# Top-1 MoE routing: all one-hot columns on VectorE, constant products in one run, and a packed table of experts

## What is computed

```python
def _moe2_ref(x, w_gate, w1, w2):          # 3072 x 512, 8 experts, hidden 1024
    logits = x @ w_gate
    expert_idx = np.argmax(logits, axis=1)
    ...
    gate_w = probs[np.arange(N), expert_idx]
    for e in range(E):
        mask = expert_idx == e
        if not mask.any():
            continue
        h = np.maximum(x[mask] @ w1[e], 0.0)
        out[mask] = gate_w[mask, None] * (h @ w2[e])
```

## Time and profile before

| | us |
|---|---|
| median of 3 runs | 458.57 |
| lowest, highest | 457.68, 459.55 |
| the profiled execution | 457.49 |
| its span in the trace | 455.8 |
| busy: TensorE, VectorE, ACT, POOL | 430.4, 237.7, 211.6, 215.1 |
| mean granted TensorE clock | 0.977 |

### The profile page before, as it was taken

The page is one execution under the profiler, slowest core; times in us unless marked ns, Lnnn a source line. Parts: engine busy times, 40 slices in busy tenths (PEclk is TensorE's granted clock), DMA queues, the critical chain, the costliest instruction groups (busy, mean ns, idle before and its releaser), DMA issues.

```text
span 455.8 us, 9239 instructions
## 1 busy us (share of the span) xinstructions
PE 430.4 (94%) x3052; PEld 359.9 (79%) x3053; DVE 237.7 (52%) x786; ACT 211.6 (46%) x417; POOL 215.1 (47%) x180
## 2 busy tenths in 40 slices
PE   8799999999999997998978959999999999999994
PEld 7699999999999996643335955688888888888883
DVE  6467777776767773557000744656433333333344
ACT  2578887878887862322010005365333333232234
POOL 3999888888888800010001156134444344443322
PEclk9989999999999998999999978999999999999998
DMA  8699998967666203999996483711111111112111
GB/s 230 260 415 372 352 366 296 399 248 269 246 214 253 81 1 111 390 387 411 396 387 206 129 313 108 283 38 58 58 58 58 58 58 58 46 46 58 53 50 13
DMA packets 27222, 89.21 MB, mean 196 GB/s; under 512 B 3280, under 2 KB 3280, under 8 KB 27184
## 3 DMA queue, kind: packets, MB, share of 16 engines
q1 hardware_dynamic: 23664, 78.47, 46.3%
q0 software_dynamic: 3360, 9.83, 7.0%
q10 hardware_dynamic: 160, 0.42, 0.5%
HBM read 80.85 MB, written 8.13 MB: 195 GB/s over the span
## 4 chain that ended last, share of the span: by engine, by line
PE 83%; DMA 5%; DVE 4%; POOL 4%; issue 1%; ACT 1%; SPq 0%; ACTq 0%; DVEq 0%; POOLq 0%
PE O L404 16%; PE Yq L1515 11%; PE Yq L1516 10%; PE Yq L1517 10%; PE PT L386 8%; PE S L377 5%; PE S L376 5%; DMA ext<-in_moe_w 4%; PE Gp L1453 3%; PE XTp L819 3%; PE Lp L938 2%; POOL work L1351 2%; PE Up L828 1%; PE Sp L1434 1%; DMA q_raw<-in_q 1%
## 5 line engine op out<-in xcount | busy, mean ns | idle before, releaser
L461 ACT ACTIVATE shared<-shared,nm 128x256 f32<-128x256 f32 (+1 forms) x192 | 83.7, 484 | 33.1 <-DVE nm L564 33.1
L404 PE MATMUL O<-V,PTs 128*128 128x65 f32 x704 | 90.9, 271 | 0.5 <-ACT PTs L487 0.5
L404 PEld LDWEIGHTS O<-V,PTs 128*128 128x128 f32 x704 | 87.4, 193 | 1.6 <-ACT PTs L487 0.9
L564 DVE CUSTOM_DVE_ANT_0 shared<-S,TA 128x256 f32<-128x256 f32 (+1 forms) x192 | 68.7, 396 | 36.9 <-PE S L377 34.2
L1515 PE MATMUL Yq<-w2h,hh 128*128 x208 | 83.2, 400 | 0.4 <-issue 0.3
L1516 PE MATMUL Yq<-w2l,hh 128*128 x208 | 81.3, 391 | 0.0
L1517 PE MATMUL Yq<-w2h,hl 128*128 x208 | 81.2, 390 | 0.0
L336 POOL TENSOR_TENSOR kl<-k_raw,kh 128x1632 fp32r<-128x1632 f32 x15 | 55.1, 3676 | 9.5 <-ACT kh L471 9.3
L1815 DVE SCALAR_TENSOR_TENSOR hl<-Gp,hh 128x512 fp32r<-128x512 f32 x56 | 38.1, 687 | 37.8 <-ACT hh L1611 37.8
L386 PE MATMUL PT<-ident,shared 128*128 128x128 f32 x352 | 55.4, 276 | 0.1
L376 PE MATMUL S<-kh,qs 128*128 128x256 f32 (+1 forms) x180 | 53.4, 319 | 1.9 <-POOL kl L336 1.9
(11 more groups left out here) (243 smaller groups left out, 583.2 us busy)
## 6 DMA issues: line engine op xcount, KB each, us to landing
mem<-in_moe_w SPq DMA_DIRECT2D x9, 2048.0 KB, 10.8
ext<-in_moe_w SPq DMA_DIRECT2D x6, 2048.0 KB, 19.4
k_raw<-in_k SPq DMA_DIRECT2D x15, 816.0 KB, 6.9
q_raw<-in_q SPq DMA_DIRECT2D x15, 768.0 KB, 5.2
V<-in_v SPq DMA_DIRECT2D x16, 715.0 KB, 4.2
xmem<-in_moe_w SPq DMA_DIRECT2D x2, 2048.0 KB, 10.5
w2l<-in_moe_w SPq DMA_DIRECT2D x2, 2048.0 KB, 13.9
w2h<-in_moe_w SPq DMA_DIRECT2D x1, 2048.0 KB, 8.3
```

The source lines that it names most:

```text
L404: mm = pe.matmul(O[grp % 2][:, at:at + VC], PTs[:, par, (h * kbs + kb) * P:(h * kbs + kb + 1) * P], V[:, buf, h, vb, :], start=(n == 0), s ...
L461: nc.scalar.activation(Pb[:, par, h, 0:width(g)], Pb[:, par, h, 0:width(g)], ACT.Exp, bias=nm[:, par, h:h + 1], scale=-1.0).then_inc(exp_d ...
L564: v.tensor_tensor_reduce(Pb[:, par, h, 0:w], S[par][h][:, 0:w], tab, -SCALE, HUGE, ALU.add, ALU.min, nm[:, par, h:h + 1]).then_inc(biased, 1)
```

## The change

1. POOL builds no columns any more. VectorE builds all six steps, behind `OA` and `OW`; `hot_first`, `places_known` and `HOTG` are gone.
2. The constant products ahead of the sort are 40 instead of 34, and the one in front of each of the last four steps is gone.
3. Units, first unit, tiles and first tile of an expert are packed in one word: VectorE computes `word` in three dependent instructions on 8 elements and multiplies it once with `sel`, where it multiplied four times. `rt` has three rows. Each engine reads one word per expert and takes it apart with shifts and masks in registers. TensorE also takes the first expert's units from the word it has, instead of a load of their own.

```diff
-    def entry(eng, r, which):
-        return eng.value_load(rt[0:1, which, bass.ds(rank_at(r), 1)], ...)
+    def plan(eng, r):
+        word = eng.value_load(rt[0:1, 1, bass.ds(rank_at(r), 1)], min_val=0, max_val=(1 << 19) - 1)
+        return ((word & 15)..., ((word >> 4) & 31)..., ((word >> 9) & 31)..., (word >> 14)...)
...
     def _(pool):
         pool.wait_ge(c_stored, 16)
-        pool.wait_ge(places_known, 1)
-        for t in range(HOTG * REP):
-            ins = nc.gpsimd.tensor_scalar(OB[:, t, :], col[:], ab[:, 1, t:t + 1], None, ALU.is_equal)
-            if t % REP == REP - 1:
-                ins.then_inc(hot_first, 1)
         pool.wait_ge(src_ready, 1)
...
-            units, first = entry(pool, rank, 1), entry(pool, rank, 2)
-            tiles, tile0 = entry(pool, rank, 3), entry(pool, rank, 4)
+            units, first, tiles, tile0 = plan(pool, rank)
...
-                    g = t // REP
-                    if g < HOTG:
-                        pe.wait_ge(hot_first, g + 1)
-                    else:
-                        if which.start == 0:
-                            busy(1)
-                        pe.wait_ge(hot_done, g - HOTG + 1)
+                    pe.wait_ge(hot_done, t // REP + 1)
...
-        busy(34)
+        busy(40)
...
-        for t in range(HOTG * REP, TT, REP):
+        for t in range(0, TT, REP):
             v.tensor_tensor(OB[:, t:t + REP, :], ..., ALU.is_equal).then_inc(hot_done, 1)
-        for i in range(2):
-            v.tensor_tensor(pick[:, 1 + 2 * i], sel[:], nt[0:1, i, :]..., ALU.mult)
-            v.tensor_tensor(pick[:, 2 + 2 * i], sel[:], begin[0:1, i, :]..., ALU.mult)
+        step(v.scalar_tensor_tensor(word[:], begin[0:1, 1, :], 32.0, nt[0:1, 1, :], ALU.mult, ALU.add))
+        step(v.scalar_tensor_tensor(word[:], word[:], 32.0, begin[0:1, 0, :], ALU.mult, ALU.add))
+        step(v.scalar_tensor_tensor(word[:], word[:], 16.0, nt[0:1, 0, :], ALU.mult, ALU.add))
+        v.tensor_tensor(pick[:, 1], sel[:], word[:]..., ALU.mult)
```

More of the change, by code:

```diff
@@ L1147, in top1_moe @@
     dst_i = sb(st, "dst_i", [P, MAXT], I32)
-    rt = sb(st, "rt", [1, 6, NE], I32)
+    rt = sb(st, "rt", [1, 3, NE], I32)
     tr = sb(st, "tr", [1, MAXU], I32)
@@ L1195, in top1_moe @@
     sel = sb(st, "sel", [1, NE, NE])
-    pick = sb(st, "pick", [1, 5, NE, NE])
-    picked = sb(st, "picked", [1, 5, NE])
+    word = sb(st, "word", [1, NE])
+    pick = sb(st, "pick", [1, 2, NE, NE])
+    picked = sb(st, "picked", [1, 2, NE])
     past = sb(st, "past", [1, MAXU, NE])
@@ L1281, in rank_at, with number @@
         return r if isinstance(r, int) else r.with_bounds(min_val=0, max_val=NE - 1)
-    def entry(eng, r, which):
-        return eng.value_load(rt[0:1, which, bass.ds(rank_at(r), 1)], min_val=int(which in (1, 3)),
-                              max_val=[NE - 1, TT // 2, MAXU - 3, TT, TT + NE - 2][which])
+    def number(eng, r):
+        return eng.value_load(rt[0:1, 0, bass.ds(rank_at(r), 1)], min_val=0, max_val=NE - 1)
+    def plan(eng, r):
+        word = eng.value_load(rt[0:1, 1, bass.ds(rank_at(r), 1)], min_val=0, max_val=(1 << 19) - 1)
+        return ((word & 15).with_bounds(min_val=1, max_val=TT // 2),
+                ((word >> 4) & 31).with_bounds(min_val=0, max_val=MAXU - 3),
+                ((word >> 9) & 31).with_bounds(min_val=1, max_val=TT),
+                (word >> 14).with_bounds(min_val=0, max_val=TT + NE - 2))
     def count(eng):
-        return eng.value_load(rt[0:1, 5, 0:1], min_val=1, max_val=NE)
+        return eng.value_load(rt[0:1, 2, 0:1], min_val=1, max_val=NE)
     def all_units(eng):
-        return eng.value_load(rt[0:1, 5, 1:2], min_val=1, max_val=MAXU - 2)
+        return eng.value_load(rt[0:1, 2, 1:2], min_val=1, max_val=MAXU - 2)
     def all_tiles(eng):
-        return eng.value_load(rt[0:1, 5, 2:3], min_val=1, max_val=TT + NE - 1)
+        return eng.value_load(rt[0:1, 2, 2:3], min_val=1, max_val=TT + NE - 1)
     def chunks_at_end(rank, used):
@@ L1322, in _ @@
         for r in range(2):
-            e = entry(sp, r, 0)
+            e = number(sp, r)
             if r:
@@ L1542, in _ @@
         used = count(pe)
-        first = halves_of(entry(pe, 0, 2))
+        units, zero = plan(pe, 0)[0:2]
+        first = halves_of(zero)
         tile(0, 0, 0, *first)
@@ L1570, in _ @@
             with pe.Fori(1, used) as rank:
-                units, first = entry(pe, rank, 1), entry(pe, rank, 2)
+                units, first = plan(pe, rank)[0:2]
                 with pe.Fori(0, units) as j:
@@ L1683, in _ @@
         with act.Fori(0, used) as rank:
-            units, first = entry(act, rank, 1), entry(act, rank, 2)
+            units, first = plan(act, rank)[0:2]
             with act.If(units > (rank < 1) * 1):
@@ L1749, in _ @@
         step(v.tensor_tensor(place[:], order[0:1, :], act[0:1, :], ALU.mult))
-        v.tensor_copy(rt[:, 5, 0:1], order[0:1, NE - 1:NE])
+        v.tensor_copy(rt[:, 2, 0:1], order[0:1, NE - 1:NE])
         step(v.tensor_tensor(sel[:], place[:].unsqueeze(1).to_broadcast([1, NE, NE]),
@@ L1767, in _ @@
         step(v.tensor_scalar(ab_i[:, 1, :], pos_i[:], P - 1, None, ALU.bitwise_and))
-        v.tensor_copy(ab[:], ab_i[:]).then_inc(places_known, 1)
-        dve.wait_ge(places_known, 1)
+        step(v.tensor_copy(ab[:], ab_i[:]))
         dve.wait_ge(c_stored, 16)
@@ L1789, in _ @@
         v.tensor_scalar(src_i[:], Sp[:, 0:MAXT], -1.0, 0.0, ALU.add, ALU.max).then_inc(src_ready, 1)
-        v.tensor_reduce(picked[:, 1:5, :], pick[:, 1:5], AX, ALU.add)
+        v.tensor_reduce(picked[:, 1, :], pick[:, 1], AX, ALU.add)
         step(v.tensor_tensor(past[:], past[:], act[0:1, :].unsqueeze(1).to_broadcast([1, MAXU, NE]), ALU.mult))
-        v.tensor_copy(rt[:, 1:5, :], picked[:, 1:5, :])
-        v.tensor_copy(rt[:, 5, 1:3], upto[0:1, :, NE - 1])
+        v.tensor_copy(rt[:, 1, :], picked[:, 1, :])
+        v.tensor_copy(rt[:, 2, 1:3], upto[0:1, :, NE - 1])
         step(v.tensor_reduce(tr_f[:], past[:], AX, ALU.add))
@@ L1878, in _ @@
         with dve.Fori(0, used) as rank:
-            units, first, tile0 = entry(dve, rank, 1), entry(dve, rank, 2), entry(dve, rank, 4)
+            units, first, _, tile0 = plan(dve, rank)
             with dve.If(units > (rank < 1) * 1):
```

8 lines of the change are left out of this document (1 added, 7 removed).

## The result

| | before | after |
|---|---|---|
| median, us | 458.38 | 450.92 (4 runs, 450.2 to 452.5) |
| ratio to before | | 0.984, 95% interval 0.981 to 0.987 |
| the profiled execution, its span | 457.49, 455.8 | 450.2, 448.5 |
| mean granted TensorE clock | 0.977 | 0.988 |

The median of before is that of all its runs by then, 458.38 where three gave 458.57. The forecast was 451.6 in a range of 449.7 to 455.4; measured were 450.92, or 7.5 us less than before where 7.0 were forecast. Step by step it is less smooth: three terms were off, and two of them cancel, which is luck.

What follows compares the result with a forecast made beforehand. TensorE was taken to bound the kernel from 304 us on, with POOL's columns in the chain before. The hidden products' gain of 7.0 us, tables counted zero, took the median 458.57 to 451.6, range 449.7 to 455.4.

Steps and rivals of the forecast that it cites:

- Columns and constants: Before the sort: six VectorE groups at 0.667 us and 40 constants in one run write src_i 6.9 us earlier.
- The gather: Behind src_i: the gather's landing sets the hidden products, 7.9 to 6.2 us earlier; the middle, 7.0, was taken.
- two prices: First gather's landing: undisturbed at 273.3, gain 7.9 us, or slowed in the issue to 275.0, gain 6.2 us.
- the row of 1.91: An earlier gather's second issue took 1.91 us while weights streamed; taken as the price of a disturbed issue.
- each step hangs on the one before as now: From the hidden products on, steps on TensorE, ACT and VectorE follow each other as before; second expert's weights covered by 2 us.
- the prediction's own sign: At the end: the prediction is wrong if the gain at the hidden products is larger than the gain at the end.
- Granted clock 1.00 from 258 to 272: Constants, sort and first fold: an expected sign that TensorE keeps its full clock throughout this stretch.
- a clock of 0.50 in 275 to 286: After the gather: a half clock in this stretch would show the prediction wrong.
- the rival on the clock: Clock falls in TensorE's new gap before the gather; takes 3.5 us off the gain, giving 455.1; chance 0.13.
- The tables: Packed tables save loads at each switch of experts, hidden under TensorE's products; counted zero, bounds -0.1 and +0.3 us.
- arrives at the end: What is won before 304 us reaches the end undiminished; what another engine wins after it is lost.
- The sum: Whole kernel: 7.0 us less, from 457.49 to 450.5 profiled and from 458.57 to 451.6 in the median.

Runs made afterwards that it cites:

- e9: The changed kernel with constant products as before: 34 in one run and one in front of each of the sort's last four steps; 451.57 us, ratio 0.984.
- e2: The kernel before with all six column groups on VectorE and 40 constant products in one run, tables not packed; 452.73 us, ratio 0.987.
- e11: The changed kernel with the first expert's last 512 KB of w2 loaded after the first gather lands, and POOL's second gather ahead of its split; 450.20 us, ratio 0.981.
- e8: The changed kernel without the unused last gather, copy and subtraction, and with POOL's quarter of the split behind the second gather and VectorE's three; 448.28 us, ratio 0.978.
- e3: The changed kernel with POOL's subtraction of the last w2 quarter moved behind the second gather and VectorE's three quarters; 450.38 us, ratio 0.983.
- e1: The kernel before with the packed tables alone, columns and constant products as they were; 457.72 us, ratio 0.998.
- e4: The changed kernel itself, run again beside other variants on the same chip; 450.85 us, ratio 0.984.
- e6: The changed kernel without the last unit's unused gather and without ScalarE's copy and VectorE's subtraction of unread weights at the end; 447.97 us, ratio 0.977.
- e10: The changed kernel once more, beside the variant with interleaved constants; 450.49 us, ratio 0.981.

## Why the prediction was right, and where it was not

- *Columns and constants.* Right: 0.61 us a group for 0.667, no wait of TensorE, the sort at full clock in 2.83 us. `src_i` is 7.4 us earlier from z, where 6.9 were forecast.
- *The gather.* The middle of two prices was taken, 7.0, and 7.2 was measured at the hidden products; neither price was the mechanism. The issue was not slowed (1.04 and 0.94), against the row of 1.91 that decided it in the prediction, and the landing was 3.0 (e9) to 3.9 us (e2) after the start of the second issue instead of 2.6: it comes with the end of the matrix (e9, e11). The rule that each DMA engine takes turns between the queues of both kinds of descriptors, "DMA: Bandwidth & Descriptors" of the Trainium skill, section "SWDGE vs HWDGE vs iDMA", would have it landed at 272.5; in the trace it was 0.9 us later. Most of its bytes seem to have moved in time (the burst at 271.50), but the landing didn't come with them. The row with 1.91 had fresh weights and a busy VectorE beside it, here there was the end of a load and an idle VectorE. Which of the two it was stays open; in e8 an issue at 277.50 took 0.94 us with both beside it (414 GB/s, VectorE's subtraction at 277.47).
- *From the hidden products on "each step hangs on the one before as now".* This step failed. The first product with `w2` came 4.16 us behind the hidden products instead of 2.46, since POOL's and VectorE's subtractions, which began 2.2 us apart before (279.71 and 281.87), now wait for the same landing and start within 0.25 us. From `hidden` to `fold 2` it is 10.88 us instead of 9.33; in e3, where the two are kept apart, 10.08. The last hidden products are 5.7 us earlier from z (6.0 in the trace's own time), where 7.0 were forecast. By the prediction's own sign it is wrong if the gain at the hidden products is larger than the one at the end: 7.2 us stand against 7.0 from z, so that sign came, if narrowly. The Trainium skill has the rule, "SBUF — State Buffer", section "Who interferes with whom": a VectorE instruction with two inputs in SBUF excludes a GpSimd instruction that reads SBUF, and the first to issue holds the port. By that rule VectorE would end at 274.12 + 2.38 + 1.22 = 277.72; the trace has 277.59. The prediction weighed this section of the Trainium skill for the gathers' descriptors only, and not for POOL's other work.
- *The clock.* "Granted clock 1.00 from 258 to 272" was wrong: 0.52 in 267.25 to 270.75, behind 11 us of unbroken work. By itself it cost little, as the fold only has to be done when the gather lands; by the order of the two subtractions it may have cost 0.5 to 1.0. The prediction blamed the low clock on TensorE's wait for POOL. The runs bear out half of this: both kernels with that wait (before, e1) have a stretch of some 10 us in the sort and first fold, and none of the twelve without has one longer than 3.5; but a stretch of 3.5 comes without the wait too. Its other sign, a clock of 0.50 in 275 to 286, did not come in after, but did in e4, the same kernel. In the rival on the clock, the middle of 1.5 and 5.0 is 3.25, not 3.5.
- *The tables.* Counted as zero with bounds of -0.1 and +0.3; they are worth 1.3 us (12.53 to 11.23) in the tail, by the traces 1.4 between e2 and e4 and 1.5 between before and e1. The term failed because "arrives at the end" was read from TensorE's unbroken chain, while the program ends with POOL's last store and its drain. That TensorE's cover hides the loads of VectorE and ACT is argued only: no run changed them alone.
- *The sum.* 5.7 + 1.3 is 7.0 from z, and 0.3 more came from the stages ahead: 7.3 of span. The forecast of 7.0 hit by an error of -1.3 and one of +1.3. That the two cancel is luck: neither the first unit nor the tail went as the prediction has it.

## To carry to other kernels

Ask which engine's list ends last, and count an engine's saved work at the end of the program even where TensorE never waits for it. When two engines' steps start to hang on the same landing, look for what they share; before the change they were apart by chance. And a transfer that is pulled ahead may be reported as landed with the end of the bulk that is queued, not after its own latency: here 512 KB less in the queue brought it forward by about 1 us, and the next transfer paid for that.

## What was not expected of the hardware

- POOL's closing drain takes 4.49 to 4.66 us, in every kernel, and starts about 2.5 to 3.1 us after its last store is issued (440.47 to 443.6 after; 439.07 to 441.6 in e6). VectorE's takes 0.3 to 0.8.
- Two `TENSOR_TENSOR` of 128x1024, on POOL and VectorE, exclude each other for their whole length: 3.2 to 3.4 us for the later one in either order.
- The granted clock went to 0.50 for about 3.5 us between 250 and 285 us in nine of the thirteen profiles behind the change (in e1 for 10 us as well), at another place in each profile of the same kernel (267.25 in after, 275.5 in e4, 268.75 in e10), also with TensorE at work throughout.
- A gather of 64 KB per issue landed 0.3 to 0.5 us behind a 2 MB load that had been issued 10 us before it, whether its second issue began 14.54 or 15.08 us from z.
